# One kernel, one core: seven raw transfers in the set-up, an inverse spread over three pairs, weight pieces and tokens at other places

## The reference, cut to what matters

```python
y[:, :, t] = einsum('bhd,bhde->bhe', rt, state)
Sa = einsum('bhde,bhe->bhd', state, at)
state = state * wt[..., None, :] - einsum('bhd,bhe->bhde', Sa, bt) + einsum('bhd,bhe->bhde', vt, kt)
```

## Time and profile before

| what | value |
|---|---|
| median of the runs (lowest to highest) | 1687.89 us (1684.33 to 1695.4) |
| the profiled execution, its own time | 1691.96 us |
| its span in the trace | 1690.3 us |
| PE busy, share of the span | 1485.6 us, 88% |
| mean granted TensorE clock | 0.946 |

### The profile page before, as it was taken

The page is one execution under the profiler, slowest core; times in us unless marked ns, Lnnn a source line. Parts: engine busy times, 40 slices in busy tenths (PEclk is TensorE's granted clock), DMA queues, the critical chain, the costliest instruction groups (busy, mean ns, idle before and its releaser), DMA issues. The chain is left out here.

```text
span 1690.3 us, 37880 instructions
## 1 busy us (share of the span) xinstructions
PE 1485.6 (88%) x15888; PEld 1295.8 (77%) x15888; DVE 810.7 (48%) x1395; ACT 421.0 (25%) x859; POOL 375.2 (22%) x314
## 2 busy tenths in 40 slices
PE   1288466998998998999997789999999999999998
PEld 0166355876877886887786669999999999999998
DVE  6876844866866776663211243333333333333333
ACT  0033233333333334323322231111111111111111
POOL 4131254333333323231132440202020202010000
PEclk9987677999999998997898989999999999999999
DMA  6544466136226316212000140100000010100011
GB/s 184 142 127 120 112 197 171 34 100 183 62 73 186 86 54 155 65 35 60 9 8 27 48 147 19 26 8 20 14 11 23 1 33 0 34 0 0 0 47 47
DMA packets 89411, 112.84 MB, mean 67 GB/s; under 512 B 10952, under 2 KB 67400, under 8 KB 89288
## 3 DMA queue, kind: packets, MB, share of 16 engines
q1 hardware_dynamic: 89288, 111.05, 23.4%
HBM read 78.73 MB, written 32.28 MB: 66 GB/s over the span
## 5 line engine op out<-in xcount | busy, mean ns | idle before, releaser
L1383 PE MATMUL banks<-x2t,u 128*128 x1536 | 377.9, 393 | 8.2 <-POOL u L1350 8.2
L1393 PE MATMUL banks<-u,hid 128*128 128x320 f32 x2304 | 360.6, 309 | 0.0
L1393 PEld LDWEIGHTS banks<-u,hid 128*128 128x128 f32 x2304 | 349.0, 188 | 11.2
L1448 DVE SCALAR_TENSOR_TENSOR hid<-banks,hid 128x512 fp32r<-128x512 f32 x192 | 132.9, 692 | 414.1 <-ACT hid L1418 414.1
L1383 PEld LDWEIGHTS banks<-x2t,u 128*128 128x128 f32 x1536 | 284.4, 189 | 61.3 <-issue 8.5
L1418 ACT ACTIVATE hid<-banks 128x512 fp32r<-128x512 f32 x192 | 115.0, 599 | 581.5 <-PE banks L1383 581.5
L814 PE MATMUL banks<-xt,wi 128*128 128x512 f32 x768 | 198.3, 401 | 19.9 <-issue 12.8
L823 PE MATMUL banks<-wo,hid 128*128 128x320 f32 x1152 | 183.8, 309 | 5.7 <-POOL hid L1220 5.7
L823 PEld LDWEIGHTS banks<-wo,hid 128*128 128x128 f32 x1152 | 175.4, 188 | 14.2 <-POOL hid L1220 6.4
L814 PEld LDWEIGHTS banks<-xt,wi 128*128 128x128 f32 x768 | 142.8, 192 | 48.1 <-issue 21.2
L1220 POOL TENSOR_TENSOR hid<-gap,hid 128x512 fp32r<-128x512 f32 x96 | 123.8, 1289 | 227.4 <-ACT hid L957 227.1
(11 more groups left out here) (105 smaller groups left out, 1552.5 us busy)
## 6 DMA issues: line engine op xcount, KB each, us to landing
scaled_operands<-made SPq DMA_DIRECT2D x42, 416.8 KB
made<-kbaw SPq DMA_DIRECT2D x42, 312.0 KB
kb<-scaled_operands SPq DMA_DIRECT2D x24, 416.0 KB
raw<-w SPq DMA_DIRECT2D x8, 640.0 KB, 5.5
lam<-scaled_operands SPq DMA_DIRECT2D x24, 209.6 KB
at<-scaled_operands SPq DMA_DIRECT2D x24, 208.0 KB
raw<-w SPq DMA_DIRECT2D x8, 512.0 KB, 4.0
rt<-rvt SPq DMA_DIRECT2D x96, 40.0 KB
```

The costliest lines, as they stand in the source:

```text
L1383: mm = pe.matmul(p_up[f][:], u1[:, par, w, f * 128:(f + 1) * 128], xt[:, x, cols], start=(i == 0), stop=(i == 7))
L1393: mm = pe.matmul(p_dn[t][:, 0:D], hid[:, f, h, t * 128:(t + 1) * 128], u2[:, par, w, f, :], start=(f == 0 and i == 0), stop=(f == NFU - 1 ...
L1448: dve.scalar_tensor_tensor(out=hid[:, f, 1, :], in0=p_up[f][:], scalar=0.0, in1=hid[:, f, 0, :].bitcast(F32), op0=ALU.max, op1=ALU.subtract)\
```

## The change

- **Set-up.** The raw transfers of the first seven units move from `start` into SP's list of the first block, ahead of the barrier. Two more slots hold the extra units; they are a new tensor `shared`, in which `nu`, `yt`, `gap` and `ut` also lie later. In `start` SP stores units 0 and 1, loads `kb` and `at` at once, then goes on; DVE masks the first scores between unit 7 and unit 8 and the second between units 8 and 9.
- **Preparation.** Four units in pair 0 and two in pair 1 (before: three and three). In pairs 0 and 1 DVE inverts the decay at once after the scan, ahead of `sides(1)`, and prepares the second unit between `sides(1)` and `sides(2)`. The last two diagonals of chunk 1 are formed in pair 1 (before: in pair 2).
- **Chunk 1's inverse.** 6 instructions at the end of pair 1, 28 in pair 2, 20 in pair 3, the last 12 after pair 3 (before: 0, 14, 14, 38).
- **Weights.** Pieces stand in pairs 2 (one), 3 and 4 (two each), 5, 6 and 7 (one each), and SP issues them ahead of the loads of `at` and `v` for the pair after the next.
- **Tokens.** The first chunk's tokens are loaded and split in pair 5, and piece 6 waits until they are split.
- **Order on PE.** `state_by_values` moves from ahead of the second answer to ahead of the fourth in pairs 0 to 2.

```diff
+EARLY = RING + 2
+PIECE_PLAN = {2: [(0, 1)], 3: [(1, 0), (2, 1)], 4: [(3, 0), (4, 1)], 5: [(5, 1)], 6: [(6, 0)], 7: [(7, 1)]}
+TOKENS_IN = 5
...
     if p < 2:
-        return list(range(FIRST + 3 * p, FIRST + 3 * p + 3))
+        return [[10, 11, 12, 13], [14, 15]][p]
...
         with nc.Block() as block:
+            @block.sync
+            def _(sp):
+                for i in range(EARLY):
+                    raw_parts(sp, i)
...
+                if p == TOKENS_IN:
+                    load_tokens(0)
+                for i, _ in pieces_in(p):
+                    raw_piece(i)
                 if p + 2 < NP:
                     load_a(p + 2)
                     load_v(p + 2)
-                if 0 <= p - PIECES_FROM < PIECES // 2:
-                    raw_piece(2 * (p - PIECES_FROM))
-                    raw_piece(2 * (p - PIECES_FROM) + 1)
...
+                if p == 1:
+                    diagonal(14)
...
+                steps = {1: (0, 0, 0, 0, 6), 2: (4, 6, 6, 4, 8), 3: (2, 2, 6, 4, 6)}.get(p, (0, 0, 0, 0, 0))
...
-                for k in i[:1]:
-                    invert_decay(k)
-                some(3)
+                if p < 2:
+                    prepare(i[1])
+                elif i:
+                    invert_decay(i[0])
+                some(1)
                 sides(2)
...
+                if p == 0:
+                    prepare(i[3])
+                elif p > 1 and i:
+                    invert_decay(i[1])
                 some(4)
                 update_state(p)
-                for k in i[2:]:
-                    prepare(k)
```

More of the change, by code:

```diff
@@ L79, in prepared_in, with pieces_in, piece_slot, pieces_in_slot @@
     if p < 2:
-        return list(range(FIRST + 3 * p, FIRST + 3 * p + 3))
+        return [[10, 11, 12, 13], [14, 15]][p]
     return [i for i in (FIRST + 2 * p, FIRST + 2 * p + 1) if i < UNITS]
 def loaded_in(p):
-    if p < 3:
-        return [[13, 14], [15], [16]][p]
+    if p < 4:
+        return [[], [15], [16, 17], [18]][p]
     return [i for i in (FIRST + 2 * p + 1, FIRST + 2 * p + 2) if i < UNITS]
+def pieces_in(p):
+    return PIECE_PLAN.get(p, [])
+def piece_slot(i):
+    return next(s for plan in PIECE_PLAN.values() for k, s in plan if k == i)
+def pieces_in_slot(i):
+    return [k for plan in PIECE_PLAN.values() for k, s in plan if s == piece_slot(i) and k <= i]
 def diagonals_before(p):
-    return FIRST + sum(len(prepared_in(k)) for k in range(p - 1))
+    return FIRST + sum(len(prepared_in(k)) for k in range(p - 1)) + (2 if p == 2 else 0)
 def tokens_turned_in(p):
-    if p == 2 * PPC - 1:
+    if p == TOKENS_IN:
         return 0
@@ L739, in start @@
             def start():
-                for i in range(8):
+                for i in range(6):
                     diagonal(i)
@@ L784, in pair @@
                 right_side_rest(p, 1, 2)
+                for i in prepared[3:]:
+                    diagonal(i)
                 if more:
@@ L794, in pair @@
                 result_by_state(p)
+                if p == 1:
+                    diagonal(15)
+                if p <= 2:
+                    state_by_values(p)
                 answer(p, 0, 3)
@@ L927, in pair @@
                 save_turned_state(p)
-                for i in prepared[1:]:
+                for i in prepared[1:3]:
                     save_diagonal(i)
@@ L932, in pair @@
                     save_answer(p, 1, b)
+                    if b == 1:
+                        for i in prepared[3:]:
+                            save_diagonal(i)
+                    if p == 1 and b == 2:
+                        save_diagonal(14)
+                        save_diagonal(15)
                 if p + 1 < NP:
@@ L1094, in start @@
                 mask_scores(0, 0)
+                prepare(8)
                 mask_scores(0, 1)
-                for i in range(8, FIRST):
-                    prepare(i)
+                prepare(9)
                 inverse_steps(0, INV_STEPS)
@@ L1126, in pair @@
                     save_result(p - 1)
-                for k in i[1:2]:
-                    scan(k, 0)
-                    scan(k, 1)
-                some(3)
+                if p == 0:
+                    prepare(i[2])
+                elif p > 1 and i:
+                    scan(i[1], 0)
+                    scan(i[1], 1)
+                some(2)
                 sides(3)
```

135 lines of the change are left out of this document (76 added, 59 removed).

## The result

| what | before | changed |
|---|---|---|
| median of 4 runs (lowest to highest) | 1689.95 us (1684.33 to 1695.4) | 1666.46 us (1664.23 to 1675.59) |
| the profiled execution: time, span | 1691.96, 1690.3 us | 1664.84, 1663.1 us |
| start of the first MLP's matmuls | 292.3 us | 264.9 us |

The median before is 1689.95 here, where the first table has 1687.89; the lowest and the highest are the same. The ratio is 0.9885 with a 95% interval of 0.9849 to 0.992: faster by 1.2% (0.8 to 1.5%). The forecast was a time of 1651, from a sum of -38.5 us over the stages; the two profiled spans differ by 27.2. The sign of the change came out, and so did the signs of the stages' terms; the gain was overrated by 11.3 us of span.

A forecast was written before the change was run, and what follows sets the result against it. PE was taken to bound the kernel from the first MLP on, but not in the first 292 us, where waits do. Stage terms sum to -38.5 us, giving 1653.5 or 1649.4; the middle, 1651, was taken, range 1637 to 1670.

The forecast's parts named there:

- Set-up: Stage before the first inverse: it would start at 48.7 us instead of 56.2, -7.5 us.
- rival A: Set-up: barrier opens only when the transfers have landed, gain 1 us instead of 7.5, time 1657.5; chance 0.12.
- Pair 1: Pair 1: 24.9 us instead of 22.7, +2.2, including a DVE wait for unit 15's raw; bounds -2 and +5.
- Pair 2: Pair 2: 28 inverse steps fill DVE's idle time nearly exactly, 21.5 us instead of 23.6, -2.1.
- Pair 3: Pair 3: 20 smaller inverse steps instead of 14, +0.6 us; bounds -2 and +3.
- After pair 3: Rest of chunk 1's inverse: 12 instructions left of 38, 6.4 us against 21.5, -15.1; bounds -17 and -13.
- I add 2.0 for two such and a short one: Stretch after pair 3: 2.0 us added for DVE steps slowed beside POOL's instructions, to the 4.4 us of before.
- Pairs 5 to 7: Pairs 5 to 7: ACT's waits for earlier-issued weight pieces go; 20.3, 20.3 and 18.6 us, -16.4 in sum.
- rival B: Transfers stay late: half of pairs 5 to 7's 16.4 us lost, pair 4 loses 3, time 1662; chance 0.18.
- The MLP's start: Start of the first MLP: piece 7's ACT and POOL instructions replace the wait for tokens, +0.4 us.
- C: Pairs 1 to 3: PE stays at the upper clock, 21, 19 and 20.5 us, -8, time 1643; chance 0.13.
- D: Pairs 3 to 7: SP blocks on a piece, operands come late, 28.2 us a pair, time 1691; chance 0.04.

The follow-up runs named there:

- e11: Changed kernel with no raw transfer ahead of the barrier, all 21 in a row behind it; 1662.87 us, one execution.
- e9: The changed kernel run once more, unedited; median of 4 runs 1663.53 us.
- e1: Changed kernel, but DVE prepares unit 15 after the masks at pair 1's end and PE forms its diagonal after the next scores; 1667.94 us.
- e10: Changed kernel with stores of units 11 and 12 in pair 0 and unit 15's raw ahead of unit 13's store; 1647.89 us.
- e7: Changed kernel with chunk 1's inverse spread as before: none in pair 1, 14 each in pairs 2 and 3, 38 after; 1670.72 us.
- e12: Changed kernel with e10, e2, e4, two raws before the barrier, unit 7's raw before `kb` and `at`, pair 4's pieces before the POOL-bound store; 1638.3 us.
- e2: Changed kernel, but POOL's weight subtractions of pair 3 wait until chunk 1's inverse is done; 1661.51 us.
- e4: Changed kernel, but PE's first MLP waits for the weights' low parts piece by piece, not for all eight; 1658.14 us.

## Why the prediction was right in kind and wrong in size

- **Set-up, -7.5 forecast, -9.6 measured.** The barrier opened with the last issue (rival A is out: the first scan stood at 11.70, not at 16), the raws were there, and the stall of 1.3 that I kept was 0.69. The units ran at 3.41 us each as priced, but for the last two, whose scans took 1.39 and 0.75 us instead of 1.71. e11 corrects the reason: the place ahead of the barrier costs as much as it brings.
- **Pair 1, +2.2 forecast, +6.9 measured, outside its bound of +5.** This is one of the two steps that failed. The step "issued at about 3.3 it lands at 7 to 9.7, and DVE waits 2 to 3" was mis-sized: the raw was issued 2.0 us into the pair but took 1.38 + 1.17 + 0.52 us to issue behind three stores, landed at about 11.8, and the wait was 5.43 (7.10 in e9), with `sides(2)` behind it. And beside it stood a wait that the sum did not have: PE's "issue" waits, read as a lack of instructions, 3.3 us here and 4.7 in e1. No wait of that kind over 0.8 us stood in the pairs of the kernel before, so I had no row for it. e10 gives the size of both as far as the order of the transfers moves them: 5.7 us.
- **Pair 2, -2.1 forecast, -2.4 measured**, and e7 shows the reason: idle DVE took the steps in.
- **Pair 3, +0.6 forecast, +2.4 measured.** DVE was busy for 18.96 of 21.4 us before; I put six more steps in and left it almost unpriced. It is now busy for 23.17 of 23.8: this pair is nearly bound by DVE (in e10 to e12, with 23.3 us of DVE and PEclk 0.73, it took 25.4).
- **After pair 3, -15.1 forecast, -10.6 measured, outside its bound of -13.** The other step that failed. The mechanism was right and the row for it was on the table; "I add 2.0 for two such and a short one" was the error. All of POOL's seven instructions fell into the stretch, because the two alternate: a DVE step waits for the POOL instruction to end, ends itself, the next POOL instruction has begun, and each side's slowness keeps the other beside it. Contention cost 5.9 us (10.9 against e2's 5.0), where the sum had 2.0. The Trainium skill's rule ("SBUF — State Buffer", section "Who interferes with whom"), by which I had counted three POOL instructions and a tail of 7.5, agrees with what the trace shows in kind; both counts were too low.
- **Pairs 5 to 7, -16.4 forecast, -14.2 measured**: 20.5, 21.7 and 19.2 against 20.3, 20.3 and 18.6. The pieces' waits did not all go: ACT waited 3.5 us in four places, PE 5.6 for ACT's diagonals. A small part of rival B: the queues moved 210 to 219 GB/s, with the 16 DMA engines 81 to 84% busy.
- **The MLP's start, +0.4 forecast, +0.6 measured.** Right, but e4 shows that about half of the gap was not needed: PE waited for the last piece to use the first.
- **Rivals.** C is out: PEclk was 0.70, 0.77 and 0.90 in pairs 1 to 3, not above 0.9. The clock doesn't set pair 1 either: it was 0.87 in e9 with the same 29.5 us, and 1.00 in the part ahead of the late raw. D is out: SP's pieces held no operand back by 10 us. B as a whole (8 us of pairs 5 to 7, 3 of pair 4) did not happen, although the median of 1666.46 lies near its number; the time agreed for another reason.
- **The number.** The sum put the profiled execution at 1653.5, and it took 1664.84: 11.3 us, the two steps above and the smaller ones. Another 2.5 come from the middle that I took towards the median of before, and 1.6 are the distance of this execution from the median of its four. The range, 1637 to 1670, holds the result. The chance of 0.93 for faster by over 1% stood on the right side, with 1.2%, but the interval of 0.8 to 1.5% doesn't exclude under 1%.

What stays open: why the packets of instructions come late in pair 1 and hardly elsewhere (e7 had one wait of 1.24 us in pair 7; the burst is supported, not isolated), what sets the granted clock of pairs 3 to 7, and what moves the stretch behind the MLP's start between 1385.5 and 1400.7 us. For the last, the same 12,280 matmuls there took 1324.87 us of PE in the changed kernel and 1315.49 in e10, and 12.6 of the 12.7 us between the two had arisen when two thirds of the first MLP's matmuls with `wi` had begun (459.6 and 447.0 us behind its start). That speaks for the granted clock (0.97 and 0.98 over the stretch); no run here sets it.

## What to carry to other kernels

When work is moved beside other work, count the whole list of the other engine that will lie there, not the instructions that lay beside it before: two engines that block each other stay side by side until one list is empty. When a wait is removed, ask what stands in the same place behind it, since a wait of 5 us may cover another of nearly 5; the cure is then the thing that both wait for, here a burst in one transfer queue. And a consumer that waits for the last piece before it touches the first (e4) is worth looking for before any reordering: a few lines moved the MLP's start by 9.2 us, a third of what the whole change had moved it. But follow the gain past the place where it is measured: five groups of matmuls later 5.4 us of it were left.
